# Attention stage of a float32 kernel on one NeuronCore: two score tiles at a time in place of one

## What is computed

```python
scores = scale * np.matmul(q, k.transpose(0, 1, 3, 2)) + bias[None]      # bias: 8 x 576 x 576, from a small MLP of positions
scores = scores - np.max(scores, axis=-1, keepdims=True)
attn = np.exp(scores)
attn = attn / (np.sum(attn, axis=-1, keepdims=True) + 1e-09)
x = np.matmul(attn, v)                                                    # then (2304, 512)
h = x @ w_in; x = (h * np.cos(h)) @ w_out                                 # d_ff 2048
xn = x / rms(x) * rms_g
out = (silu(xn @ w_gate) * (xn @ w_val)) @ w_out2                          # d_ff 1536
```

## Time and profile before

| | |
|---|---|
| median of 3 runs | 1207.83 us (1207.55 to 1208.03) |
| the profiled execution's own time | 1208.74 us |
| its span | 1207.0 us |
| PE busy in the span | 1171.1 us (97%) |
| DVE, ACT, POOL busy | 704.4, 496.3, 490.4 us (58%, 41%, 41%) |
| attention, first to last score tile and its end | about 68 to 341 us |

### The profile page before, as it was taken

One profiled execution on the slowest core, in us unless ns is written; L12 is line 12 of the kernel. 1 busy time (PEld: TensorE's weight loads), 2 busy tenths in 40 slices (PEclk: granted clock), 3 DMA queues, 4 the chain that ended last, 5 costly groups with the idle time before them and its releaser, 6 DMA issues. The chain is left out here.

```text
span 1207.0 us, 21829 instructions
## 1 busy us (share of the span) xinstructions
PE 1171.1 (97%) x7464; PEld 1078.6 (89%) x7464; DVE 704.4 (58%) x1540; ACT 496.3 (41%) x1034; POOL 490.4 (41%) x515
## 2 busy tenths in 40 slices
PE   5789999999989999999999999999999999999998
PEld 2267777777779999999999999999999999999998
DVE  8978888888889867777786887553011020210201
ACT  6967787787723433333343333111111111111111
POOL 3047777777766342525243362751111111111111
PEclk9989999999999999999999999999999999999999
DMA  5754535252144000000000011330000000000000
GB/s 172 247 174 126 170 99 170 100 188 81 56 114 123 18 2 1 0 0 0 0 0 0 0 36 35 105 114 27 1 1 26 0 26 0 0 26 0 26 0 26
DMA packets 46534, 69.06 MB, mean 57 GB/s; under 512 B 3712, under 2 KB 27424, under 8 KB 46496
## 3 DMA queue, kind: packets, MB, share of 16 engines
q1 hardware_dynamic: 46496, 68.60, 18.3%
HBM read 53.25 MB, written 15.34 MB: 57 GB/s over the span
## 5 line engine op out<-in xcount | busy, mean ns | idle before, releaser
L820 PE MATMUL banks<-x_high,w_low_rest 128*128 128x384 f32 x672 | 224.5, 334 | 0.0
L818 PE MATMUL banks<-x_high,w_high_rest 128*128 128x384 f32 x672 | 224.4, 334 | 0.0
L819 PE MATMUL banks<-x_low,w_high_rest 128*128 128x384 f32 x672 | 224.4, 334 | 0.0
L1367 DVE TENSOR_TENSOR X<-X,banks 128x384 f32<-128x384 f32 x72 | 39.8, 552 | 298.6 <-PE banks L820 298.5
L1386 POOL TENSOR_TENSOR product_low<-X,product_high 128x384 fp32r<-128x384 f32 x72 | 72.8, 1012 | 345.5 <-ACT product_high L1329 345.5
L1184 POOL TENSOR_TENSOR product_low<-g,product_high 128x384 fp32r<-128x384 f32 x96 | 102.3, 1066 | 236.9 <-ACT product_high L1066 236.9
L818 PE MATMUL bank<-product_high,w_high_rest 128*128 128x384 f32 x480 | 162.1, 338 | 0.8 <-POOL product_low L1184 0.8
L820 PE MATMUL bank<-product_high,w_low_rest 128*128 128x384 f32 x480 | 160.5, 334 | 0.0
L819 PE MATMUL bank<-product_low,w_high_rest 128*128 128x384 f32 x480 | 160.5, 334 | 0.0
L1094 ACT ACTIVATE angle<-angle,quarter 128x384 f32<-128x384 f32 x96 | 59.3, 617 | 201.9 <-DVE angle L1126 201.9
L644 DVE CUSTOM_DVE_ANT_0 probs<-banks,bias 128x576 f32<-128x576 f32 (+1 forms) x160 | 119.7, 748 | 20.6 <-PE banks L506 10.0
(11 more groups left out here) (113 smaller groups left out, 2525.4 us busy)
## 6 DMA issues: line engine op xcount, KB each, us to landing
raw_qk<-in_qk SPq DMA_DIRECT2D x32, 576.0 KB, 3.8
bias_scratch<-bias_stage SPq DMA_DIRECT2D x36, 288.0 KB, 3.2
bias<-bias_scratch SPq DMA_DIRECT2D x32, 288.0 KB, 3.4
w_raw<-in_w_out SPq DMA_DIRECT2D x28, 256.0 KB, 2.7
values<-in_v SPq DMA_DIRECT2D x16, 320.0 KB, 4.1
w_raw<-in_w_in SPq DMA_DIRECT2D x16, 256.0 KB, 2.9
out_t<-X SPq DMA_DIRECT2D x5, 768.0 KB, 3.6
w_raw<-in_w_gate SPq DMA_DIRECT2D x12, 256.0 KB, 3.3
```

Source lines behind the costliest of these rows:

```text
L818: nc.tensor.matmul(out, high, x_high, start=start, stop=False)
L819: nc.tensor.matmul(out, high, x_low, start=False, stop=False)
L820: return nc.tensor.matmul(out, low, x_high, start=False, stop=stop)
```

## The change

On every engine the slots are taken two by two. PE scores tiles `s` and `s + 1`, then turns the tiles 4 back from both, then does a piece of the mix; the pieces stand in double slots 4, 6, 8 and 0, so that double slot 2 has none. ACT makes two copies, then two exponentials. DVE does the reduction of `s`, `guard` and `invert` of `s - 1`, the reduction of `s + 1`, `normalise` of `s - 2`, and `guard` and `invert` of `s`. `keep_end` moves from behind slot 3 to behind double slot 4, and `keep_mixed` of the first half from behind slot 5 to behind double slot 6. POOL's and SP's lists are unchanged. No instruction is added or taken away.

```diff
-MIX_SLOTS = (3, 5, 8, 0)
+MIX_SLOTS = (4, 6, 8, 0)
...
-            def slot(n, parity, s, step, compute=True):
+            def slots(n, parity, s, step, compute=True):
 
                 if compute:
                     score(n, s, step == 0)
-                if s < T_LAG:
-                    if step > 0:
-                        turn(n - 1, TILES - T_LAG + s, False)
-                elif compute:
-                    turn(n, s - T_LAG, step == 0)
+                    score(n, s + 1, step == 0)
+                for r in (s, s + 1):
+                    if r < T_LAG:
+                        if step > 0:
+                            turn(n - 1, TILES - T_LAG + r, False)
+                    elif compute:
+                        turn(n, r - T_LAG, step == 0)
                 if s == MIX_SLOTS[3]:
...
-                for s in range(TILES):
-                    slot(n, parity, s, step)
+                for s in range(0, TILES, 2):
+                    slots(n, parity, s, step)
...
-                for s in range(TILES):
-                    if s >= T_LAG:
-                        keep(n, parity, s - T_LAG)
-                    elif not first:
-                        keep(n - 1, 1 - parity, TILES - T_LAG + s)
+                for s in range(0, TILES, 2):
+                    for r in (s, s + 1):
+                        if r >= T_LAG:
+                            keep(n, parity, r - T_LAG)
+                        elif not first:
+                            keep(n - 1, 1 - parity, TILES - T_LAG + r)
                     exps(n, s)
+                    exps(n, s + 1)
...
+            def sum_inverse(n, parity, step, s):
+                m, _, r = back(n, parity, s, EXP_LAG)
+                if s >= EXP_LAG or step > 0:
+                    guard(m, r)
+                    invert(m, r)
...
-                    if s >= EXP_LAG or step > 0:
-                        guard(m, r)
-                    if (s >= EXP_LAG + 1 or step > 0) and r3 not in POOL_TILES:
-                        normalise(dve, m3, r3, dve_normed)
-                    if s >= EXP_LAG or step > 0:
-                        invert(m, r)
-                    if step > 0 and s == T_LAG - 1:
+                    sum_inverse(n, parity, step, s)
+                    if hp is not None:
+                        dve.wait_ge(att.bias_in[s + 1], (hp + 1) * 16)
+                    add_bias(n, s + 1, step == 0)
+                    if s >= EXP_LAG + 1 or step > 0:
+                        normalise(dve, m2, r2, dve_normed)
+                    sum_inverse(n, parity, step, s + 1)
+                    if step > 0 and s == T_LAG:
                         keep_end(n - 1, 1 - parity)
```

More of the change, by code:

```diff
@@ L580, in _ @@
                 pair(m * 2 + 1, 1, 2)
-            for s in range(MIX_SLOTS[1] + 1):
-                slot(PAIRS, 0, s, 2, compute=False)
+            for s in range(0, MIX_SLOTS[1] + 1, 2):
+                slots(PAIRS, 0, s, 2, compute=False)
             pe.wait_ge(biased, PAIRS * TILES)
@@ L669, in back @@
                 return (n, parity, s - by) if s >= by else (n - 1, 1 - parity, TILES + s - by)
+            def sum_inverse(n, parity, step, s):
[3 more added lines that the diff above has]
+                    invert(m, r)
             def pair(n, parity, step, hp=None):
-                for s in range(TILES):
-                    m, _, r = back(n, parity, s, EXP_LAG)
-                    m3, _, r3 = back(n, parity, s, EXP_LAG + 1)
+                for s in range(0, TILES, 2):
+                    m2, _, r2 = back(n, parity, s, EXP_LAG + 1)
                     if hp is not None:
```

## The result

The changed kernel takes **1215.49 us** (1215.35 to 1216.06) against 1207.87 us beside it: a ratio of 1.006, 95% interval 1.0047 to 1.0074, so 7.6 us slower. The forecast was 1219.0 us, in a range from 1210.5 to 1229. The profiled execution took 1216.06 us with a span of 1214.3, 7.3 more than before.

What follows compares the result with a forecast made beforehand. The prediction took PE to bound the kernel. It summed 0.70 us a pair over fifteen pairs (10.5), 0.4 and 0.3 to +11.2 us, 1219.9 for an execution like the profiled one, so 1219.0 us; range 1210.5 to 1229.

Steps and rivals of the forecast that it cites:

- The exits of the 64-row shape: On PE, leaving the 64-row transposes of tiles 4 and 9 costs 0.20 each, +0.40 us a pair, bounds 0 and 0.56.
- The sign that I had named for it: In PE's timeline after: the first matmul behind the 64-row transposes starts 0.15 to 0.25 late.
- Tile 5's scores wait for reduction 3: In double slot 2: these scores come 0.1 late, part of +0.30 us a pair for waits.
- Tile 0's transposes late: Behind double slot 2: they wait for DVE's normalisation, 0.05 to 0.55 late.
- the 0.30: Waits on PE around double slot 2, +0.30 us a pair, 0.2 at best and 0.65 at worst.
- Pairing scores and transposes saves nothing: On PE: twenty changes between scores and transposes per pair become ten, which saves 0.
- The first pair and the end: First pair pays its 64-row exits, 0.4 us; at the end tile 7's transposes move ahead of a mix, 0.3 us.
- DVE becomes the bound: Rival, chance 0.20: normalisations take 0.99 on average, DVE needs 17.6 us a pair against 16.32, total about 1228 us.
- this rule: DVE and POOL share a locked port pair: a normalisation starting behind POOL's long pass waits for all of it.
- ACT's list costs nothing: ACT's new order adds no time, since ACT is idle for 3.4 us a pair in waits for PE.
- Faster: Rival, chance 0.07: PEld's 8.8 us idle is a real wait of scores behind a mix and goes: 1197 us.
- The clock falls: Rival, chance 0.02: longer transpose runs lower the granted clock, 8 us a pair, total above 1300 us.

Runs made afterwards that it cites:

- e4: The kernel before with only the mix slots changed, to 4, 6, 8 and 0 from 3, 5, 8 and 0: 1210.65 us, ratio 1.0023.
- e2: The changed kernel with tile 5 turned and copied ahead of tile 4, whose 64-row transposes then stand directly ahead of the mix: 1217.43 us, ratio 1.0077.
- e6: The changed kernel with a double slot's two reductions next to each other on DVE, guard and reciprocal behind the second: 1218.93 us, ratio 1.009.
- e5: The changed kernel with DVE back in its one-tile order, the copies of mix and tail staying where the changed kernel has them: 1218.83 us, ratio 1.0093.
- e9: The kernel before with only ACT's work in the new order, two copies and then two exponentials: 1213.07 us, ratio 1.0036.
- e1: The changed kernel with the mix pieces in double slots 2, 6, 8 and 0 in place of 4, 6, 8 and 0: 1218.26 us, ratio 1.0089.
- e7: The kernel before with the mix's 128-column end matmul replaced by two of 64 columns, one for each head: 1207.5 us, ratio 0.9997.

## Why the prediction was right

- **The exits of the 64-row shape**, +0.40 a pair: right. 0.20 towards scores, as taken, and 0.15 towards transposes, 0.35 together; by themselves in e4 (0.19) and e2 (0.14). The sign that I had named for it was too coarse: the first matmul behind them starts 0.09 late, and the rest of the price stands between it and the second.
- **Tile 5's scores wait for reduction 3**: right in place and releaser; 0.20, half of it in front of the first score matmul and half between it and the second. The chain ran 0.2 later than laid out, since the first two score matmuls behind the end matmul are 0.35 apart (219.57, 219.92) and not 0.13. Reduction 2 started 0.52 behind the last score of its tile (220.18, 220.70), as laid out, but so 1.13 behind the slot's first score and not 0.92, and reduction 3 at 2.27 and not 2.04. The copy of the mix, which DVE has ahead of it, had ended at 220.55. One link I had not seen is the buffer: reduction 3 may not start ahead of tile 8's transposes (e6).
- **Tile 0's transposes late**, the rest of the 0.30: wrong, they never were. The normalisation ended 3.48 behind the slot's start (222.53 + 0.52) and the transposes came at 3.74, because the wait before tile 5 had already put them off; without its 0.20 they would have come at 3.54, still behind it. I added two waits of one chain, of which the first hides the second. With the exits at 0.35 for 0.40 this made 0.70 out of what is 0.57.
- **Pairing scores and transposes saves nothing**: right; all of the 0.57 is accounted for without it.
- **The first pair and the end**, +0.4 and +0.3: wrong in sign, -0.8 and -0.3. The first goes with the granted clock at the start of attention, 0.76 here and 0.54 before, which differs from kernel to kernel. With the fourteen periods at 0.57 in place of fifteen at 0.70, the terms come to +7.0 and not +11.2; the medians are 7.6 apart. So the forecast is right by its mechanism on PE and by the width of its range, not by its small terms.
- **DVE becomes the bound**: refuted. Its normalisations became shorter, 575 ns for 714, and POOL's longer; DVE is left 2.8 us a pair idle, where the layout left 0.7. The Trainium skill, SBUF — State Buffer, section "Who interferes with whom", says that issue order decides who blocks. The trace agrees as far as the means go: the turn between the two changed, and the cost went from DVE to POOL, which sits idle for 45.0 us ahead of its normalisations. The pair of instructions that I had read for this rule fits in size alone. POOL's, which took 1.16, is the one that started first (220.51), and DVE's, behind it, took its shortest time:

```profile
220.63 0.50 DVE L412 TENSOR_SCALAR probs<-probs,inv_total 128x576 f32<-128x576 f32 x1
```

  Which of the two was issued first no trace here shows, so the rule stays unproven in this kernel.
- **ACT's list costs nothing**: right by the trace, though not for its slack. The guard now waits for it 11.2 us in 200, but neither of the two reductions of the chain does (see e5); alone, in PE's old order (e9), it cost 4 us.
- **Faster**: refuted. The row of PEld's idle time fell from 8.8 us to 2.5 and nothing was gained, for it was hardly a wait of PE's: its own distances before scores hold 0.02 us a pair of waiting in the kernel before.
- **The clock falls**: refuted, 1.00 from 106.4 to 333 us.

## What to carry to other kernels

When PE has no idle time, count the changes of its weights' shape, and put one shape change where another is paid anyway: 64-row transposes directly ahead of a mix cost nothing extra, ahead of 128-row transposes 0.15 us and ahead of scores 0.20. Where engines hand tiles to each other, an order is a property of all of them: DVE's new order cost 51 us on the old order of PE and gained 3 us on the new one, though DVE was idle a sixth of the time in the kernel before and in the changed one. Before queueing a wait, ask which instruction stands behind it and who waits for that; copies queued one or two places too early cost 34 us.

## What was not expected of the hardware

- Over a change of shape a weight load starts with its matmul (221.94 for both) where between two scores it runs 0.13 us ahead; that is seen in every such exit of both traces. From 128-row transposes to scores, in the kernel before, it runs 0.03 ahead.
- The granted clock fell at the end of attention in e2, to 0.72 over 342 to 348 us, and in e9, to 0.73 over 340.6 to 346.6 us. It did not in the changed kernel, whose attention differs from e2's only in the order of two tiles, nor in e1, after PE had been busy for 2.35 of 4 us, nor in e7, after 2.24 of 4 (331.4 to 335.4 us); in e9 it had been 2.27 (336.6 to 340.6 us). The fall cost e2 about 1.6 us; what decides it stays open.
